# Expert weights loaded from ScalarE's queue behind the first regular gather, in a recurrence + two-MoE kernel

## The reference

```
for t in range(768):                       # linear recurrence, 4 batches x 8 heads, head width 48
    y[:, :, t] = r_t . (state + (u * k_t) v_t^T)
    state = w * state + k_t v_t^T
h = max(x @ w1, x @ w2, x @ w3);  x = h @ w_out            # 384 -> 768 -> 384
noisy = x @ w_gate + log1p(exp(x @ w_noise)) * noise       # 8 experts
top2, weights = softmax over the two largest of noisy
for e in range(8):                                          # 384 -> 1024 -> 384
    out[mask] += weight * (relu(x[mask] @ w1[e]) @ w2[e])
```

## Time and the profile before

| | |
|---|---|
| median of 3 runs | 980.56 us (980.24 to 982.49) |
| profiled execution | 977.49 us, of which its span is 975.6 us |
| PE busy | 931.2 us (95% of the span) |
| DVE, ACT, POOL busy | 458.3, 256.2, 432.1 us |
| mean granted clock of PE | 0.983 of full speed |
| DMA | 85.02 MB, mean 87 GB/s |

### The profile page before, as it was taken

The page is one execution under the profiler, slowest core; times in us unless marked ns, Lnnn a source line. Parts: engine busy times, 40 slices in busy tenths (PEclk is TensorE's granted clock), DMA queues, the critical chain, the costliest instruction groups (busy, mean ns, idle before and its releaser), DMA issues.

```text
span 975.6 us, 18718 instructions
## 1 busy us (share of the span) xinstructions
PE 931.2 (95%) x6410; PEld 926.4 (95%) x6411; DVE 458.3 (47%) x993; ACT 256.2 (26%) x462; POOL 432.1 (44%) x408
## 2 busy tenths in 40 slices
PE   4799999999999999999979989999999999999996
PEld 4699999999999999999969989999999999999996
DVE  7555264636646474654533434253443435252322
ACT  1242221311222131323321431242312224141211
POOL 5445443635444263543533445353443443534343
PEclk9699999999999999999989989999999999999999
DMA  7467211212121121003261331515151525312122
GB/s 174 116 188 226 64 34 59 57 42 55 51 57 40 58 57 32 25 0 93 79 171 42 113 96 57 176 43 183 37 188 56 176 79 174 88 47 69 42 78 64
DMA packets 94959, 85.02 MB, mean 87 GB/s; under 512 B 51994, under 2 KB 84450, under 8 KB 94912
## 3 DMA queue, kind: packets, MB, share of 16 engines
q1 hardware_dynamic: 72816, 53.94, 19.2%
q0 software_dynamic: 12096, 25.69, 8.7%
q10 hardware_dynamic: 10000, 4.82, 1.7%
HBM read 69.55 MB, written 21.15 MB: 93 GB/s over the span
## 4 chain that ended last, share of the span: by engine, by line
PE 44%; DMA 4%; issue 2%; DVE 1%; POOL 1%; POOLq 0%; DVEq 0%; ACT 0%; ACTq 0%; SPq 0%
PE ps L1303 14%; PE ps L1304 14%; PE ps L1305 14%; PE ps L1342 2%; DMA xg<-x_rows,ent_e 1%; DMA prev<-out,ent 1%; DMA out<-yrow,ent 1%; DMA ent<-lists 1%; DMA e_raw<-ew 0%; POOL lists L495 0%; DMA xg<-x_rows,ent 0%; DVE w1l L928 0%; POOL prev L597 0%; POOLq L87 0%; DVE yrow L1020 0%
## 5 line engine op out<-in xcount | busy, mean ns | idle before, releaser
L1303 PE MATMUL ps<-xgh,w1h 128*128 128x256 f32 (+1 forms) x648 | 182.8, 282 | 1.7 <-DVE xgl L994 1.1
L1305 PE MATMUL ps<-xgh,w1l 128*128 128x256 f32 (+1 forms) x648 | 182.8, 282 | 0.0
L1304 PE MATMUL ps<-xgl,w1h 128*128 128x256 f32 (+1 forms) x648 | 182.7, 282 | 0.0
L1303 PE MATMUL ps<-yh,wh 128*128 128x384 f32 x432 | 148.4, 344 | 4.3 <-ACT hmax L1107 1.7
L1197 ACT ACTIVATE gh<-ps 128x512 fp32r<-128x512 f32 x108 | 64.3, 597 | 320.1 <-PE ps L1305 310.5
L1304 PE MATMUL ps<-yl,wh 128*128 128x384 f32 x432 | 145.5, 337 | 0.0
L1305 PE MATMUL ps<-yh,wl 128*128 128x384 f32 x432 | 145.5, 337 | 0.0
L597 POOL DMA_INDIRECT prev<-out,ent x50 | 59.5, 1190 | 188.7 <-DMA ent<-lists 181.1
L1303 PE MATMUL ps<-w2h,gh 128*128 128x384 f32 x408 | 140.1, 343 | 0.3 <-DVE gl L999 0.3
L1304 PE MATMUL ps<-w2l,gh 128*128 128x384 f32 x408 | 137.5, 337 | 0.0
L1305 PE MATMUL ps<-w2h,gl 128*128 128x384 f32 x408 | 137.3, 337 | 0.0
(11 more groups left out here) (172 smaller groups left out, 1688.4 us busy)
## 6 DMA issues: line engine op xcount, KB each, us to landing
ew_raw<-ew SPq DMA_DIRECT2D x28, 768.0 KB, 7.2
v_sb<-vN SPq DMA_DIRECT2D x24, 192.0 KB, 2.6
wraw<-moe_w SPq DMA_DIRECT2D x8, 576.0 KB, 4.8
out<-zrow SPq DMA_DIRECT2D x1, 4608.0 KB, 17.4
x_rows<-x_sb ACTq DMA_DIRECT2D x8, 576.0 KB, 3.5
kn_sb<-kN SPq DMA_DIRECT2D x20, 192.0 KB, 2.7
k_raw<-kT SPq DMA_DIRECT2D x48, 72.0 KB, 1.9
r_raw<-rT SPq DMA_DIRECT2D x48, 72.0 KB, 2.0
```

The costliest lines, as they stand in the source:

```text
L1303: pe.matmul(o, ah, bh, start=start, stop=False)
L1304: pe.matmul(o, ah, bl, start=False, stop=False)
L1305: return pe.matmul(o, al, bh, start=False, stop=stop)
```

## The change

`load_expert` moves from SP to ACT. The load of expert 1 is issued by ACT after its evictions of tile g = 1, once the first regular gather (tile g = 2) has landed, and ahead of `turn_rows(2)`. The load of expert e + 2 is issued by ACT at the end of its part of expert e, behind the entry load of that expert's last tile, once expert e + 1 is split. SP loads entries alone, in one loop over the tiles of each expert. PE's one wait for all evictions of x ahead of the first products is replaced by waits ahead of the first three products that use banks 0, 1 and 2, each for the eviction of that bank.

```diff
-            def load_expert(e):                       # on SP
-                for q in range(NPE):
-                    if not known(e, 2):
-                        sp.wait_ge(ewh_ok, NPE * (e - 1) + q + 1)
-                        sp.wait_ge(ewl_ok, NPE * (e - 1) + q + 1)
-                    ...
-                    sp.dma_start(ew_raw[:, q * PIECE:(q + 1) * PIECE], ...).then_inc(ew_in, 16)
-            def load_first(first, m0): ...
-            def load_others(first, n, m0): ...
+            def load_entries(first, n, m0):
+                with sp.Fori(0, n) as t:
+                    sp.wait_ge(xg_in, 32 * (m0 + t + EARLY))
+                    sp.dma_start(ent[:, :, :], lists[bass.ds(first + t * T, T), :]...).then_inc(entG_in, 16)
...
-            sp.wait_ge(x_mm, BS * NBLK)
-            load_expert(1)
             sp.wait_ge(plan_ok, 1)
             sp.wait_ge(x_stored, 16 * NBLK)
             sp.wait_ge(listed, 16 * 2 * BS * (NBLK + 1))
-            load_first(first, m0)
-            load_others(first, n, m0)
-            with sp.Fori(1, NE - 1) as e:
+            with sp.Fori(0, NE - 1) as e:
                 n, m0, first = expert_plan(e)
-                load_first(first, m0)
-                load_expert(e + 1)
-                load_others(first, n, m0)
+                load_entries(first, n, m0)
...
+            def load_expert(e):                       # on ACT
+                for q in range(NPE):
+                    act.dma_start(ew_raw[:, q * PIECE:(q + 1) * PIECE], ...).then_inc(ew_in, 16)
...
+                if load_next:                         # at the end of ACT's expert(e, ...)
+                    act.wait_ge(ewl_ok, NPE * (e + 2))
+                    load_expert(e + 2)
...
             for q in range(4):
                 high_rows(1, q)
+            act.wait_ge(xg_in, 16 * TS * (EARLY + 1))
+            load_expert(1)
             turn_rows(2)
...
-                if g == 0:                            # PE, early(g)
-                    pe.wait_ge(x_ok, BS * NBLK)
                 for f in range(F2T):
+                    if g == 0 and f < 2 * BS and f % 2 == 0:
+                        pe.wait_ge(x_ok, BS * (NBLK - 1) + f // 2 + 1)
                     first_product(g, 0, f, T)
```

More of the change, by code:

```diff
@@ L362, in _ @@
                 sp.dma_start(e0_raw[q % 2][:, :], src[0, :, at:at + PIECE]).then_inc(e0_in[q % 2], 16)
-            def load_expert(e):
-                for q in range(NPE):
-                    if not known(e, 2):
-                        sp.wait_ge(ewh_ok, NPE * (e - 1) + q + 1)
-                        sp.wait_ge(ewl_ok, NPE * (e - 1) + q + 1)
-                    src, at = (ew1, q * PIECE) if q * PIECE < W1P else (ew2, q * PIECE - W1P)
-                    sp.dma_start(ew_raw[:, q * PIECE:(q + 1) * PIECE],
-                                 src[bass.ds(e, 1), :, at:at + PIECE].rearrange("a p n -> (a p) n")).then_inc(ew_in, 16)
-            def load_first(first, m0):
-                sp.wait_ge(xg_in, 32 * (m0 + EARLY))
-                sp.dma_start(ent[:, :, :], lists[bass.ds(first, T), :].rearrange("(s p) w -> p s w", p=P)).then_inc(entG_in, 16)
-            def load_others(first, n, m0):
-                with sp.If(n > 1):
-                    with sp.Fori(1, n) as t:
-                        sp.wait_ge(xg_in, 32 * (m0 + t + EARLY))
-                        sp.dma_start(ent[:, :, :], lists[bass.ds(first + t * T, T), :].rearrange("(s p) w -> p s w", p=P)
-                                     ).then_inc(entG_in, 16)
+            def load_entries(first, n, m0):
+                with sp.Fori(0, n) as t:
+                    sp.wait_ge(xg_in, 32 * (m0 + t + EARLY))
+                    sp.dma_start(ent[:, :, :], lists[bass.ds(first + t * T, T), :].rearrange("(s p) w -> p s w", p=P)
+                                 ).then_inc(entG_in, 16)
             def expert_plan(e):
@@ L1209, in tile, with expert @@
                     split_high(1 - par, 0, NPE, ew_raw, 0)
-            def expert(e, par, split_next):
+            def expert(e, par, split_next, load_next):
                 n = act.value_load(plan[0:1, 0, bass.ds(e, 1)], min_val=1, max_val=NTOK // T)
@@ L1233, in _ @@
                 for par in range(2):
-                    expert(2 * m + par, par, True)
-            expert(NE - 2, 0, True)
-            expert(NE - 1, 1, False)
+                    expert(2 * m + par, par, True, True)
+            expert(NE - 2, 0, True, False)
+            expert(NE - 1, 1, False, False)
         @block.tensor
```

7 lines of the change are left out of this document (4 added, 3 removed).

## The result

The changed kernel took 973.62 us (median of 9 executions, 972.74 to 977.55) against 979.41 us of the kernel before in the same comparison (9 executions, 976.19 to 984.53, the three of before's first measurement among them). The ratio is 0.9942, 95% interval 0.9923 to 0.9962: faster by 5.8 us, where 14.4 were forecast. So the sign was right and less than half of the gain came. 973.62 lies inside the range of 963.5 to 974.0, at its upper end; the likeliest value, 966.2, is 7.4 us off. That it lies inside is luck: the upper end was drawn for rival B, whose stall did not happen. Later comparisons of the same two kernels gave ratios from 0.9867 to 0.9960, and that spread is a result of its own.

A forecast was written before the change was run, and what follows sets the result against it. PE, busy 95% of the span, was taken as the bound, together with its stalls. Gains of 0.7 + 7.9 + 6.6 = 15.2 us less 0.8 make 14.4, from the median 980.56 to 966.2 us; range 963.5 to 974.0.

The forecast's parts named there:

- rival B: Gather of tile 5 under expert 2's load: second stall stays in size, only 8.6 us gained, 972.0 us; chance 0.14.
- What is late next?: Behind the early gather: DVE's rank step and list writes move earlier, first regular gather lands at 520.9, 2.3 us to spare.
- tile 3: Its gather falls into expert 1's load, takes 5.4 us where 5.1 are allowed: cost 0.3, bounds 0 and 1.9.
- The first stall: PE's wait for the second early gather: without expert 1's load at 489 it goes, 6.2 + 1.7 = 7.9 us gained.
- The 0.7 us for x: PE's wait for an x eviction ahead of its first products: finer waits remove it, gain 0.7 us.
- the whole give-back of 4.0: Time lost again to gathers under the moved loads: 0.3 + 0.3 + 0.2 = 0.8 us, bounds 0 and 4.0.
- The second stall: PE's wait for a regular gather, tile 5, 4.2 + 2.4 = 6.6 us: 6.3 gained, gather taking 5.4 to 7.0.
- Tile 8: Half tile ending expert 1, gather under a load: 6.0 us allowed; costs 0.2 with 6.2, 1.0 with 7.0.
- ACT's new wait and its issues: ACT's wait for the first regular gather and four issues ahead of turn_rows(2): cost 0, cover 0.7 us.
- SP's single loop: SP's entry loads: only takes waits for splits from between entries; PE waits for no entry load, so nothing.
- C: Slower: every x gather under a load takes 12.1 us, 25.1 lost against 15.2, 990.5 us, break-even 10.5; chance 0.08.
- D: Early gather is slow through x store and list writes, not the load: about 979 us; chance 0.05.

The follow-up runs named there:

- e5_after_fourth: The changed kernel, unchanged, run again beside two versions with SP's plan read ahead: 964.48 us, 0.9867 of the kernel before.
- e2_before_again: The kernel before, unchanged, run again for a second profile: 976.53 us, ratio 1.0005.
- e1_one_x_wait: The changed kernel with PE's one wait for all x evictions put back: 971.95 us, 0.9948 of the kernel before.
- e2_no_later_loads: The changed kernel without the loads of experts 2 to 7, computed with expert 1's weights (output differs): 963.0 us, 0.9865 of the kernel before.
- e5_plan_ahead: The changed kernel with SP reading expert 0's plan ahead of its waits for stored rows and lists: 963.7 us, 0.9866 of the kernel before.
- e1_expert1_alone: The kernel before with only expert 1's load moved to ACT, later loads and the x wait as before: 974.67 us, 0.9968.
- sets 1 and 4: Comparisons of the kernel before (977.16 and 978.2 us) with the changed kernel and parts of the change, and with expert 1's load alone and ACT's issue behind turn_rows(2).
- sets 2, 3 and 5: Comparisons with the kernel before (976.24, 975.05, 978.28 us): later loads dropped or on SP, early scatter moved; ACT's code written out; SP's plan read ahead.
- e4_expert1_again: Repeat of the kernel before with only expert 1's load moved to ACT: 976.3 us, 0.9993 of the kernel before.
- e1_x_waits_alone: The kernel before with the finer waits of PE on x and nothing else: 976.91 us, 0.9998.
- e4_before_third: The kernel before, unchanged, run again for a third profile: 978.51 us, ratio 1.0003.
- e3_after_third: The changed kernel, unchanged, run again: 963.79 us, 0.9902 of the kernel before.
- e3_after_unrolled: The changed kernel with ACT's experts 0 and 1 written out ahead of its loop, all loads still on ACT: 965.43 us, 0.9899 of the kernel before.

## Why the prediction was right and where it failed

The sign held, and both stalls went as forecast; the size failed, 5.8 us in place of 14.4. The step that failed is the one behind "What is late next?": it looked at DMAs and DVE, found "2.3 us to spare" and booked the early stages with the whole 0.7 + 7.9 = 8.6 us. In the profile of after they gave 2.1, because PE's own first banks reached ACT 4.2 and 4.3 us late. The second fault is the base: the stalls of one execution of before, 6.2 and 4.2 us, were taken for the kernel's.

Two accounts, both against the first profile of before, on which the sum was made. In `e5_after_fourth` the stretch gained 11.7 of the 14.4 us: short were 0.6 in the early stages (8.0 of 8.6), 0.6 at tile 2 (forecast 0), 0.7 from turn 4 to 6 (5.6 of 6.3) and 1.1 at tile 8 (a loss of 1.3, forecast 0.2); tile 3 gave back nothing, where 0.3 were forecast. In the profile of after it gained 6.4: the early stages gave 2.1 of 8.6, which is 6.5 of the 8.0 that are missing. That term is the one that failed most.

**The first stall: "The whole wait goes, and with it the half clock: 6.2 + 1.7 = 7.9."** The wait for the gather went in every version without SP's early load. "What is late next?" was then asked of DMAs and DVE only, and late next was a completion of PE's own first bank, by 4.2 us, with a route wait of 1.5 us and 3.4 us at half clock behind it. Where completions were not late, the term was right against before's first profile: 8.0 us with the 0.7 of the x wait in it (6.1 against `e2_before_again`). The 0.7 us for x are not shown by themselves: the finer waits alone gave nothing (0.9998), where late completions and the early gather, which they don't touch, hold PE behind them; `e1_one_x_wait` has the 0.7 us wait back, without a loss in the median. The medians go the same way: in sets with late completions the whole change gave 5.8 us (0.9942) and 3.2 (977.16 less 973.98), in the others 11.3 (975.05 less 963.79) and 13.8 (978.28 less 964.48). From 980.56 us those two ratios, 0.9902 and 0.9867, would give 970.9 and 967.5, beside the 966.2 of the forecast.

**The base: one execution's stalls taken as the kernel's.** The sum subtracts 6.2, 4.2 and their clock from the earlier trace rows. Two more profiles of the same program had 4.3 and 2.7, and 0.9 and 2.9. By the table the stretch of before varies by 5.2 us, more than the whole give-back of 4.0 for which I had set bounds; the range had no room for it.

**The second stall: "of 4.2 + 2.4 = 6.6 us I get 6.3 back."** Mechanism right, sizes off on both sides. The gather of tile 5 took 6.40 us (568.00) in after, between the 5.4 and 7.0 that I took as bounds, but PE waited 1.04 us for it, and 0.4, 1.2 and 1.3 us in the other profiles of after, where 0.3 were forecast (none in two of the three profiles with two loads on ACT, 1.2 in the third). No clock fell, as forecast. The stretch from turn 4 to turn 6 took 18.4 + 19.9 = 38.3 us in before's first profile and 14.7 + 17.8 = 32.5 in after: 5.8 of the 6.3. Against `e2_before_again` (35.2) it is 2.7: this term too depends on which execution of before one looks at.

**Tile 8: "with 6.2 it costs 0.2."** The gather took 7.46 us, over the 7 that I had named as a sign of being wrong; PE waited 1.53, and 1.1 to 1.4 us in the other traces of after. `e2_no_later_loads` and all versions that keep the loads of experts 3 to 7 on SP lose this wait (13.5 us for the stage in place of 15.0), so it is the load above the gather: shown. The full tiles cost nothing, as forecast (329 us from turn 9 to the end in every kernel). The waits given back at the loads thus sum to 2.6 us in after (1.04 + 1.53) where 0.8 were forecast; the bound of 4.0 held.

The Trainium skill (DMA: Bandwidth & Descriptors, "Queues, rings and completion order") has each DMA engine take turns between the queues that have work. The trace bears it out only in part: gathers under a load took 6.4 and 7.5 us against 3.0 alone, so they were slowed less than the 12.1 us of before, but did not land as if alone. With the Trainium skill (DMA: Bandwidth & Descriptors, "Issuing engines are not separate DMA queues": the transfers of all issuing engines share the same DMA engines) the traces agree: gathers issued by POOL were slow under a load that SP issued (12.1 us in before) and under loads that ACT issued (6.4 and 7.5 us in after).

**"ACT's new wait and its issues ... Cost 0, cover 0.7 us. If the gather is 1 us later than I think, 0.3 us show."** The rule was right. In the profile of after the cover held: the issues ended at 530.82, PE's turning began at 531.15, and the wait for `xgl` stayed at 1.1 us, since late completions had put PE behind. In the profiles without them the condition came true. The four issues took 2.0 to 2.4 us (2.1 to 2.3 forecast), and the gather was 2.2 us later than need be, so the wait rose from 1.1 us to 1.4 to 2.0.

**"SP's single loop only takes SP's waits for splits from between entries. ... so nothing."** Wrong. The single loop also moved the reading of the plan behind SP's last wait: the entry load went out 2.7 us behind the wait, 2.2 us later than with the plan read ahead, on the path to the first regular gather. `e5_plan_ahead` shows the link to PE's wait; its price, 0.6 us, is below what the medians can tell.

**The rivals.** B (the second stall stays) gives 972.0, closer to the result than the forecast, for a wrong reason: that stall went, and late completions took most of the gain of the first. C (every gather under a load takes 12.1 us) fell: they took 6.4 and 7.5, under its break-even of 10.5. D (the load was not the cause) fell: without the load the early wait is gone in each trace, `e1_expert1_alone` among them, which moves nothing else.

**What stays open** is the cause of the late completions. They came with the set (in all seven profiles of sets 1 and 4, before among them, in none of sets 2, 3 and 5) and not with the chip: one chip gave set 1 and set 3. The packed traces of such executions hold 9,151 to 9,437 semaphore records where those of the others hold 11,433 to 11,453 (11,067 without the later loads), so the recording itself may be part of it; but the medians of the executions without a profile follow the kind of the set (973.9 and 974.5 against 963.9 and 964.4). The profiles show 2.5 to 5.9 us of these 10 in the early stages, and more ahead of the change: after (972.82) against `e5_after_fourth` (964.57), with the same clock at first, is 8.3 us, of which 5.3 lie in the stretch and 2.7 in the first part. In before the medians hardly follow the kind (977.2 and 978.2 against 976.2, 975.1 and 978.3), since there the stall of the early gather hides part of it. Loading of code is not the cause as far as the traces tell: in both kinds the first transfers on the instruction queues around this place lie about 7 and 5 us ahead of the first products of tile 0, and the next comes 10 us or more behind them. That the scatter in flight causes them was tried only in a set that had none; it is neither shown nor refuted.

## What to carry to other kernels

Before a stall is booked as a gain, look at it in more than one execution of the kernel: here it was 6.2, 4.3 and 0.9 us in three profiles of one program, and other waits stood behind it. When a loop is merged, count the register reads that its head puts behind the last wait, as one counts DMAs. And a transfer moved away from one victim has a new one: write down for each moved load which gather now lies under it and how many microseconds that gather may take.

## What was not expected of the hardware

- ACT began to evict the first bank 1.8 to 4.9 us after its last matmul in the two early tiles of after and of all seven profiles of sets 1 and 4, idle for most of that time; in the eleven other profiles it followed at once or about 0.5 us later, behind its own step for the route chain. In the profile of after PE itself stood 0.85 us in the same place.
- The clock fell to 1.2 GHz at 501.4 after stops of 0.85 and 1.53 us (ended at 497.72 and 500.36), and stayed there until 504.8; single stops of 1.0 to 1.5 us at tiles 5 and 8, the 2.7 us of `e2_before_again` and the 3.4 us of `e4_expert1_again`, cost no clock. A stop of 2.9 us cost none in `e1_x_waits_alone` and was followed by 6.8 us at half clock in `e4_before_third` (0.50 from 580 to 586). The length of the stop alone does not tell.
- Three reads of the plan on SP behind a wait moved its next DMA 2.2 us back, and the four DMA issues of expert 1 on ACT took 2.0 to 2.4 us (once 2.8), in line with its evictions.
- Between executions without late completions the start of the second part moves by 8 us (485.8 to 494.2), more than most effects here. Much of it stands by 100 us: ACT's first eviction of x is at 99.8 us in `e3_after_third` (clock 0.87 from 20 to 60 us) and at 104.7 in `e3_after_unrolled` (0.74). The latter also had 0.91 from 100 to 120 and 0.93 from 460 to 486 us.
